# Seven block products for the first layer of three quarters of a dense network, on one Trainium2 core

## The reference

```python
def _moe_ref(x, U, V, w_ch1, w_ch2):          # x: 2 x 768 x 512
    xt = x.transpose(0, 2, 1)
    h = xt @ U @ V
    u = x + h.transpose(0, 2, 1)
    ch = np.maximum(u @ w_ch1, 0.0) @ w_ch2   # 512 -> 2048 -> 512
    return u + ch
```

## Time and profile before

| | us |
|---|---|
| median of 3 runs | 510.38 |
| lowest, highest | 510.18, 510.39 |
| the profiled execution | 510.51 |
| its span, first to last instruction | 508.7 |
| TensorE busy | 501.7 |
| VectorE busy | 255.3 |
| ScalarE busy | 202.3 |
| GpSimd busy | 45.6 |

### The profile page before, as it was taken

How to read it: one execution, slowest core, us unless ns; L and a number is a source line. 1 busy time by engine, 2 the same in 40 slices (tenths; PEclk the granted TensorE clock), 3 DMA queues, 4 the chain that set the end, 5 groups by cost and what they waited for, 6 DMA issues and landing times.

```text
span 508.7 us, 8626 instructions
## 1 busy us (share of the span) xinstructions
PE 501.7 (99%) x3460; PEld 468.5 (92%) x3460; DVE 255.3 (50%) x594; ACT 202.3 (40%) x403; POOL 45.6 (9%) x65
## 2 busy tenths in 40 slices
PE   8899999999999999999999999999999999999997
PEld 7679999999999999999999999999889889989987
DVE  5776654655455345354453554785544643552501
ACT  6575531442433244241431413554723632551410
POOL 6693310301000000000000000000000000000000
PEclk9999999999999999999999999999999999999999
DMA  8998533112112022132231331300010000001001
GB/s 283 339 267 265 150 110 92 43 44 83 41 44 82 1 84 62 36 134 100 79 130 41 126 125 43 124 1 1 0 43 21 2 27 36 0 15 48 1 0 62
DMA packets 13127, 40.53 MB, mean 80 GB/s; under 512 B 1728, under 2 KB 2240, under 8 KB 13088
## 3 DMA queue, kind: packets, MB, share of 16 engines
q1 hardware_dynamic: 12656, 39.20, 24.0%
q10 hardware_dynamic: 432, 0.79, 0.4%
HBM read 36.84 MB, written 3.15 MB: 79 GB/s over the span
## 4 chain that ended last, share of the span: by engine, by line
PE 94%; DMA 3%; POOL 1%; DVE 0%; SPq 0%; issue 0%; POOLq 0%
PE ps L788 91%; DMA V<-in_V 3%; PE ps L843 2%; PE ps L791 1%; DMA vT<-in_vT 1%; POOL Vs L370 1%; POOL vwin L386 0%; DVE vsum L593 0%; POOL Vs L366 0%; SPq L245 0%; DVE scratch L781 0%; SPq L208 0%; SPq L220 0%; DVE mixr L626 0%; DVE mixr L624 0%
## 5 line engine op out<-in xcount | busy, mean ns | idle before, releaser
L788 PE MATMUL ps<-u_hi,w_hi 128*128 128x384 f32 x256 | 87.4, 341 | 0.0
L788 PE MATMUL ps<-h_hi,w_hi 128*128 128x384 f32 x256 | 87.1, 340 | 0.0
L788 PE MATMUL ps<-h_hi,w_lo 128*128 128x384 f32 x256 | 85.9, 335 | 0.0
L788 PE MATMUL ps<-h_lo,w_hi 128*128 128x384 f32 x256 | 85.9, 335 | 0.0
L788 PE MATMUL ps<-u_hi,w_lo 128*128 128x384 f32 x256 | 85.9, 335 | 0.0
L788 PE MATMUL ps<-u_lo,w_hi 128*128 128x384 f32 x256 | 85.8, 335 | 0.0
L507 ACT ACTIVATE h_hi<-ps 128x384 fp32r<-128x384 f32 x64 | 31.5, 492 | 118.2 <-PE ps L788 118.1
L704 DVE SCALAR_TENSOR_TENSOR h_lo<-ps,h_hi 128x384 fp32r<-128x384 f32 x64 | 35.7, 558 | 68.6 <-ACT h_hi L507 68.5
L709 DVE TENSOR_TENSOR yT<-ps,yT 128x384 f32<-128x384 f32 x64 | 35.6, 556 | 54.1 <-PE ps L788 54.1
L788 PEld LDWEIGHTS ps<-u_hi,w_hi 128*128 128x128 f32 x256 | 48.1, 188 | 1.8 <-issue 1.5
L788 PEld LDWEIGHTS ps<-h_hi,w_hi 128*128 128x128 f32 x256 | 48.0, 188 | 1.5 <-issue 1.5
(11 more groups left out here) (96 smaller groups left out, 752.2 us busy)
## 6 DMA issues: line engine op xcount, KB each, us to landing
wraw<-in_w SPq DMA_DIRECT2D x42, 512.0 KB, 3.5
vwin<-in_vw SPq DMA_DIRECT2D x7, 580.5 KB, 13.1
kT<-in_kT SPq DMA_DIRECT2D x8, 400.0 KB, 8.8
vT<-in_vT SPq DMA_DIRECT2D x8, 384.0 KB, 10.0
out<-scratch SPq DMA_DIRECT2D x11, 256.0 KB, 2.0
qt<-in_qT SPq DMA_DIRECT2D x6, 384.0 KB, 11.7
vwin<-in_vw SPq DMA_DIRECT2D x1, 387.0 KB, 8.4
qt<-in_qT ACTq DMA_DIRECT2D x1, 384.0 KB, 7.0
```

The costliest lines, as they stand in the source:

```text
L788: return nc.tensor.matmul(o, lhsT, rhs, start=start, stop=stop)
```

## The change

Quarters 5, 6 and 7 do the first layer by Strassen's scheme in Winograd's form. The hidden block pair and the feature pairs make a 2x2 block matrix of the weights (feature halves i by hidden halves f, blocks of 256x256), the features and token chunks a 2x2 block matrix of u. Seven products of blocks take the place of eight. For each j (0, 1: the 128-wide half of a hidden block) there is one pair index m = 2(Q-5) + j and seven products, each of 6 matmuls 128x384, in the order P1, P6, P7, P5, P2, P4, P3, in banks 3 to 7 in turn.

- GpSimd forms four sums of u (T1 to T4, 128x768) after u is complete, and for each fast quarter four sums of w1 (S1 to S4, 128x512) from `wraw`. High and low halves of these: ScalarE and VectorE (`high_t`, `low_t` at g = 4, 6 of Q=4; `high_s`, `low_s` at g = 12, 13 of Q=4 and after the drains of k = 3, 5 of the second layers).
- VectorE forms seven sums from the products' banks (x, y, c22, z, c11, c21, c12), ScalarE copies P1 out. The hidden rows come from SBUF sums: h rows 0, 1 from c11, 2, 3 from c21, 4, 5 from c12, 6, 7 from c22. ScalarE writes all high halves; low halves of c11 and c21 are VectorE's, of c22 and c12 GpSimd's, in two instructions each.
- The second layer keeps its 96 matmuls; its first group waits for the low halves of c11 and c21.
- SyncE's w2 parts of quarters 5 to 7 wait for the third and fourth sum of GpSimd. The m2 parts are spread anew: two in Q=4, two in Q=5, none in Q=6, two in Q=7's second layer, four in the final stage's first eight groups.
- Buffers for the sums lie over those of the attention; m2's buffers are in two pieces.

```diff
@@ -40,7 +40,12 @@
...
-PARTS_LAST = [(1, "w2", 0), (3, "w2", 1), (4, "m2", 0), (6, "m2", 1), (7, "m2", 2), (9, "m2", 3)]
+S1, S3, S2, S4 = range(4)
+T1, T2, T4, T3 = range(4)
+NP = 7
+P1, P6, P7, P5, P2, P4, P3 = range(NP)
+LATE_AT = [0, 1, 4, 5]
+PREV_W2 = [-2, -4, -1, 0, 1, 2, 3, 5]
 UX_SLOT, XV_SLOT = 50, [52, 56]
@@ -179,14 +201,31 @@
         def parts_before(b, Q):
-            return 4 * Q + 2 if b == 0 else 6 * Q - 6
+            return 4 * Q + 2 if b == 0 else (18, 24, 30, 34)[Q - 4]
@@ -280,13 +319,14 @@
                 n += 1
                 load_part(n, src)
             for r in range(NQ):
-                last = r == NQ - 1
                 parts = [w2_part(r, 0), w2_part(r, 1)]
-                parts += [m2_part(m) for m in (range(2 * r, 2 * r + 2) if not last else range(6, 10))]
-                if not last:
+                parts += [m2_part(m) for m in ((0, 1), (2, 3), (), range(4, 10))[r]]
+                if r < NQ - 1:
                     parts += [w1_part(r + 1, a) for a in range(2)]
-                for src in parts:
+                for j, src in enumerate(parts):
                     n += 1
+                    if r > 0 and j < 2:
+                        sp.wait_ge(s_step, 4 * (r - 1) + 3 + j)
                     load_part(n, src)
             out_rows = out.rearrange("b s c -> (b s) c")
@@ -430,6 +470,56 @@
...
+                nc.gpsimd.tensor_tensor(two(t_sum, n, CH), a, b, op).then_inc(t_step, 1)
+            def u_block(i, c):
+                return yT[:, 1, 2 * i:2 * i + 2, 1 + CH * c:1 + CH * c + CH]
+            pool.wait_ge(yt_done, 16)
+            pool.wait_ge(ulo_done, 12)
+            t_add(T1, u_block(0, 1), u_block(0, 0), ALU.subtract)
+            pool.wait_ge(t_step, 1)
+            t_add(T2, u_block(1, 1), two(t_sum, T1, CH), ALU.subtract)
+            pool.wait_ge(t_step, 2)
+            t_add(T4, u_block(1, 0), two(t_sum, T2, CH), ALU.subtract)
+            t_add(T3, u_block(1, 1), u_block(0, 1), ALU.subtract)
+            def s_add(n, a, b, op):
+                nc.gpsimd.tensor_tensor(two(s_sum, n, 256), a, b, op).then_inc(s_step, 1)
+            def w_sums(q):
+                def w_block(i, f):
+                    return wraw[:, i, :].rearrange("p (t n) -> p t n", t=2)[:, :, 256 * f:256 * f + 256]
+                n = parts_before(1, Q=5 + q)
+                pool.wait_ge(w_in[0], 8 * n)
+                pool.wait_ge(w_in[1], 8 * n)
+                if q == 0:
+                    pool.wait_ge(tlo_done, 2)
+                need(pool, slo_done, 2 * q)
+                s_add(S1, w_block(0, 1), w_block(1, 1), ALU.add)
+                s_add(S3, w_block(0, 0), w_block(0, 1), ALU.subtract)
+                pool.wait_ge(s_step, 4 * q + 1)
+                s_add(S2, two(s_sum, S1, 256), w_block(0, 0), ALU.subtract)
+                pool.wait_ge(s_step, 4 * q + 3)
+                s_add(S4, w_block(1, 0), two(s_sum, S2, 256), ALU.subtract)
+            def low_relu(row, src, order, m, done):
+                pool.wait_ge(hb_done, 4 * m + order)
+                nc.gpsimd.tensor_scalar(src, src, 0.0, None, ALU.max).then_inc(relu_sums, 1)
+                pool.wait_ge(relu_sums, 2 * m + (1 if order == 1 else 2))
+                nc.gpsimd.tensor_tensor(h_lo[:, row, :], src, h_hi[:, row, :].bitcast(f32), ALU.subtract).then_inc(done, 1)
+            w_sums(0)
+            for q in range(3):
+                for j in range(2):
@@ -528,15 +618,10 @@
...
+                        high_t((g - 4) // 2)
+                    if b == 1 and g in (12, 13):
+                        high_s(0, g - 12)
             def mix_scale(b, c, p, n):
@@ -555,14 +640,71 @@
                     if p > DC * i:
                         mix_high(p - 1, n0 + p - 1)
+            def high_t(i):
+                act.wait_ge(t_step, 2 * i + 2)
+                nc.scalar.activation(t_hi[:, 2 * i:2 * i + 2, :], t_sum[:, 2 * i:2 * i + 2, :], ACT.Copy).then_inc(thi_done, 1)
+            def high_s(q, i):
+                act.wait_ge(s_step, 4 * q + 2 * i + 2)
+                act.wait_ge(pr_done, 14 * q)
+                nc.scalar.activation(s_hi[:, 2 * i:2 * i + 2, :], s_sum[:, 2 * i:2 * i + 2, :], ACT.Copy).then_inc(shi_done, 1)
+            def high_part(Q, i, kind, j):
+                n = parts_before(1, Q) + i + 1
+                act.wait_ge(w_in[(n - 1) % 2], 16 * ((n + 1) // 2))
+                nc.scalar.activation(part_dst(kind, j, 1, Q, True), wraw[:, (n - 1) % 2, :], ACT.Copy).then_inc(whi_done, 1)
+            def relu_sum(row, src):
+                nc.scalar.activation(h_hi[:, row, :], src, ACT.Relu).then_inc(hb_done, 1)
+            def fast_quarter(Q):
+                q = Q - 5
+                for j in range(2):
+                    m = 2 * q + j
...
+                    need(act, c11_sum, m)
+                    nc.scalar.activation(summed("p1"), p_bank(m, P1), ACT.Copy).then_inc(p1_copied, 1)
+                    if j == 0:
+                        high_part(Q, 0, "w2", 0)
+                    elif Q == 5:
+                        high_part(Q, 2, "m2", 0)
+                    act.wait_ge(c22_sum, m + 1)
+                    relu_sum(6 + j, summed("c22"))
+                    act.wait_ge(c11_sum, m + 1)
+                    relu_sum(j, summed("c11"))
+                    if j == 0:
+                        high_part(Q, 1, "w2", 1)
+                    elif Q == 5:
+                        high_part(Q, 3, "m2", 1)
+                    act.wait_ge(c21_sum, m + 1)
+                    relu_sum(2 + j, summed("c21"))
+                    act.wait_ge(c12_sum, m + 1)
+                    relu_sum(4 + j, summed("c12"))
+                if Q < 7:
+                    for i in range(2):
+                        high_part(Q, (4 if Q == 5 else 2) + i, "w1", i)
+                    for i in range(2):
+                        high_s(q + 1, i)
@@ -727,13 +871,84 @@
...
+            def low_relu(row, src, order, m, done):
+                dve.wait_ge(hb_done, 4 * m + order)
+                nc.vector.scalar_tensor_tensor(out=h_lo[:, row, :], in0=src, scalar=0.0, in1=h_hi[:, row, :].bitcast(f32),
+                                               op0=ALU.max, op1=ALU.subtract).then_inc(done, 1)
...
+            def add_to(out, product, other, m, done):
+                dve.wait_ge(pr_done, NP * m + product + 1)
+                nc.vector.tensor_tensor(summed(out), p_bank(m, product), summed(other), ALU.add).then_inc(done, 1)
+            def fast_quarter(Q):
+                q = Q - 5
+                for j in range(2):
+                    m = 2 * q + j
+                    dve.wait_ge(p1_copied, m + 1)
+                    need(dve, h11_done, m)
+                    add_to("x", P6, "p1", m, x_sum)
+                    if j == 0:
+                        low_part(Q, 0, "w2", 0)
+                    elif Q == 5:
+                        low_part(Q, 2, "m2", 0)
+                    dve.wait_ge(x_sum, m + 1)
+                    need(dve, h21_done, m)
+                    add_to("y", P7, "x", m, y_sum)
+                    dve.wait_ge(y_sum, m + 1)
+                    need(dve, h22_done, m)
+                    add_to("c22", P5, "y", m, c22_sum)
+                    need(dve, h12_done, m)
+                    add_to("z", P5, "x", m, z_sum)
+                    dve.wait_ge(z_sum, m + 1)
+                    add_to("c11", P2, "p1", m, c11_sum)
+                    dve.wait_ge(c22_sum, m + 1)
+                    add_to("c21", P4, "y", m, c21_sum)
+                    low_relu(j, summed("c11"), 2, m, h11_done)
+                    add_to("c12", P3, "z", m, c12_sum)
+                    low_relu(2 + j, summed("c21"), 3, m, h21_done)
+                    if j == 0:
+                        low_part(Q, 1, "w2", 1)
+                    elif Q == 5:
+                        low_part(Q, 3, "m2", 1)
+                for k in range(8):
+                    c, d = divmod(k, DC)
+                    dve.wait_ge(dense_done, 80 + 8 * q + k + 1)
+                    nc.vector.tensor_tensor(x_out(1, d, c), bank(BANK[8 + k], CH), x_out(1, d, c), ALU.add).then_inc(drained, 1)
+                    if Q < 7:
...
+                        if k in (0, 2):
+                            low_part(Q, (4 if Q == 5 else 2) + k // 2, "w1", k // 2)
+                        if k in (3, 5):
+                            low_s(q + 1, (k - 3) // 2)
+                    else:
+                        for p in (k,) if k < 7 else (7, 8):
+                            if p < 8:
+                                mix_add(0, 0, p, p)
+                            if p > 0:
+                                mix_low(p - 1, p - 1)
+                        if k in (1, 4):
@@ -756,12 +971,15 @@
             for Q in range(NQ):
                 quarter(0, Q, PARTS_B0)
-            for Q in range(NQ, 2 * NQ):
-                quarter(1, Q, PARTS_B1 if Q < 7 else PARTS_LAST)
+            quarter(1, 4, PARTS_B1)
+            for Q in range(5, 8):
```

(75 more changed lines are left out.)

85 lines of the change are left out of this document (64 added, 21 removed).

## The result

The changed kernel takes 509.44 us (median of 12 runs, 508.43 to 513.02), beside 510.99 of the kernel before on the same chips (12 runs, 510.18 to 513.14): a ratio of 0.9972, 95% interval 0.9959 to 0.9986, some 1.5 us or 0.3% faster. Repeated with 12 more runs it was 0.9980 (0.9965 to 0.9994). The forecast was 506.1, 4.3 us faster. The sign was right, the size nearly three times too large.

A forecast was written before the change was run, and what follows sets the result against it. TensorE, busy 99% of the span, was taken as the bound. Removed matmuls 6.24, less stalls 1.68 and final-stage lag 0.15, gave 4.41 us off the profiled 510.51: 506.1 us, range 504.1 to 510.0.

The forecast's parts named there:

- The saving: First layers of Q=5 to 7: 84 matmuls instead of 96 each, at 0.1733 us, 6.24 us less.
- The place of the stall: One TensorE gap of 0.5 to 0.7 us a quarter, at the second layer's first matmul; none at P6.
- I take 0, the row's own behaviour, and keep the other end: VectorE starting during GpSimd work: cost per meeting 0 to 0.93 us, taken as 0 from a copy at 59.02 us.
- the walk: Operation-by-operation timing of the product pairs: stalls 1.68 us before the second layers; total 504.7 to 507.5 us, chance 0.56.
- the second: VectorE waits 0.46 us at each operation with two SBUF inputs: 509.2 us; chance 0.23 including mild forms of late sums.
- The third: VectorE and GpSimd exclude each other wholly in the product pairs, bounding TensorE through the banks: 517.0 us; chance 0.08.
- The fourth: GpSimd's s sums late at P6, 2.4 us each instead of 1.2: 512.6 us; chance 0.05 in full.
- the fifth: TensorE loses an interval to waits at each of 42 products, 7.1 us, nothing left: 513 us; chance 0.02.
- the first: Handovers cost nothing or the timing of the pairs is too slow: 504.1 us, the floor; chance 0.06.
- Handovers: From the end of a VectorE operation to the restart of a stalled TensorE's matmul: 0.29 us.
- GpSimd's durations: GpSimd low half in the pairs: max of some 0.45 us plus 0.93 subtraction, 1.5 with the handover.
- The final stage: Four m2 parts in its first 8 groups: lag 3.8 against 3.6 us slack at second value group, costing 0.15.

The follow-up runs named there:

- both edits: Changed kernel plus GpSimd's second-pair low halves waiting for VectorE's c11 half and second-layer hidden rows in order 0, 2, 1, 3: 505.97 us, 0.9904.

## Why the prediction was right or wrong

**The saving: right.** 36 matmuls of 0.1733, 6.24 us, are gone, and where nothing else waits (Q=6, both edits) 14.59 stands for 16.64.

**The place of the stall: right.** One wait a quarter, at the second layer's first matmul, released by VectorE's low half; no stall at a product, none at P6 (the second s half ends at 240.28 and 272.39, wanted near 242.4 and 274.9), none through the four late parts.

**Its size: wrong, and this is the step that failed.** The sum had 0.72 + 0.48 + 0.48 = 1.68; it is 1.23 + 1.34 + 1.35 = 3.92, 2.24 more. The failing step is the sentence on VectorE beginning while GpSimd is at work, "I take 0, the row's own behaviour, and keep the other end". In the row at 59 us VectorE came first. When it comes second, it waits: in Q=6 and Q=7 the half of c11 comes second, because GpSimd's c22 subtraction has just begun, and in Q=5 the weight parts ahead of it do. The runs price it: 0.65 in Q=5 (15.79 to 15.14 without GpSimd's halves), 0.80 and 0.81 in Q=6 and 7 (15.90 and 15.91 to 15.10 with GpSimd moved behind), 2.26 in all. What is left is 0.58, 0.54 and 0.54, 1.66, against the walk's 1.68. That the sums agree to 0.02 is luck (the walk had 0.72, 0.48 and 0.48, 0.14 too much in Q=5 and 0.06 too little twice), but no quarter is off by more than 0.14. The walk was sound; a known unknown was entered at its cheap end, 0, where the other end that the prediction names, 0.93, was near the 0.8 measured. In Q=5 the meetings lie earlier, at the parts (VectorE, then GpSimd):

```profile
249.50 0.73 DVE L898 SCALAR_TENSOR_TENSOR h_lo<-c_sum,h_hi 128x384 fp32r<-128x384 f32 x1
250.16 1.52 DVE L892 TENSOR_TENSOR w_lo<-wraw,w_hi 128x1024 fp32r<-128x1024 f32 x1
251.61 0.54 DVE L903 TENSOR_TENSOR c_sum<-ps,c_sum 128x384 f32<-128x384 f32 x1
252.07 1.57 DVE L892 TENSOR_TENSOR m2a_lo<-wraw,m2a_hi 128x1024 fp32r<-128x1024 f32 x1
253.57 2.66 DVE L903 TENSOR_TENSOR c_sum<-ps,c_sum 128x384 f32<-128x384 f32 x5
256.36 0.56 DVE L898 SCALAR_TENSOR_TENSOR h_lo<-c_sum,h_hi 128x384 fp32r<-128x384 f32 x1
...
250.08 1.19 POOL L511 TENSOR_SCALAR c_sum<-c_sum 128x384 f32<-128x384 f32 x1 [0.26 <-ACT h_hi L658]
251.35 1.22 POOL L513 TENSOR_TENSOR h_lo<-c_sum,h_hi 128x384 fp32r<-128x384 f32 x1
```

The two parts take 1.52 and 1.57, not 1.22, and the half of c21 ahead of them 0.73; counted from the start of Q=5, the half of c11 at 256.36 comes 0.64 later than in the kernel without GpSimd's halves. The second part waited to near the end of GpSimd's subtraction (252.57). The first came 0.08 after the start of a max of 1.19 and lost only 0.30. So beside a max the wait is not its whole length, and it is the same each time: over the ten traces 31 operations of VectorE came early in a max, and all really began 0.80 to 0.81 us before its end, 0.35 to 0.39 after its start, while ten that came later than that lost nothing. Why a max lets go so early is open.

**The rivals.** The measured 509.44 stands next to the 509.2 of the second, and that is luck. It had the mechanism, VectorE waiting, and the wrong place for it: I charged it to VectorE's total, which gave 3.1 in Q=5 and nothing in Q=6 and 7 because there was time to spare. But the price is paid by the one operation that TensorE waits for, or by those right ahead of it in VectorE's order, spare time or not, so that it is nearly even over the quarters (0.65, 0.80, 0.81). The third, full exclusion bounding TensorE through the banks, did not come. Between two-input operations the exclusion is nearly whole, but GpSimd is idle when most of VectorE's come, and the PSUM adds don't meet it. The fourth (late sums), the fifth (intervals lost at the products) and the first (504.1) are out.

**Handovers.** Forecast 0.29 from the end of VectorE to TensorE's matmul; measured 0.25, and then another 0.08 to the second matmul of the row. Three times 0.08 are the 0.25 of the repeated profile that the sum did not have; the first profile's 0.49 has intervals longer by some 0.0013 us through the second layers of Q=6 and Q=7 besides.

**GpSimd's durations.** "a max of some 0.45 (from the cast)" was far too low (min/median/max in ns over the changed kernel):

```profile
L511 POOL TENSOR_SCALAR c_sum<-c_sum x12: 1165/1168/2256, 247.1 to 323.4; 128x384 f32<-128x384 f32 x12
...
L513 POOL TENSOR_TENSOR h_lo<-c_sum,h_hi x12: 1012/1201/1572, 248.4 to 324.6; 128x384 fp32r<-128x384 f32 x12
```

A max of 128x384 takes 1.17, 2.26 when VectorE holds it up. The h12 rows had time for it, but it also moved GpSimd's subtraction under the half of c11. An estimate from the rows of Q=6: with a max of 0.45 from 286.85 and the same 0.08 between the two, the subtraction would have run from 287.38 to 288.39, and the half of 288.18 would have lost some 0.07 and not 0.79. So two terms failed together in Q=6 and Q=7: the wait that was put at nothing, and the duration that brought the meeting about. No run separates them, as none has a shorter max.

**The final stage.** Forecast: lag 3.8 against 3.6 of slack, 0.15. VectorE's second s half for Q=5 and for Q=6, ScalarE's last copy of the first chunk and its first gates in the changed kernel:

```profile
239.07 1.21 DVE L886 TENSOR_TENSOR s_lo<-s_sum,s_hi 128x1024 fp32r<-128x1024 f32 x1
...
271.17 1.22 DVE L886 TENSOR_TENSOR s_lo<-s_sum,s_hi 128x1024 fp32r<-128x1024 f32 x1 [0.69 <-ACT s_hi L650]
...
360.59 0.53 ACT L711 ACTIVATE h_hi<-scratch 128x384 fp32r<-128x384 f32 x1 [0.71 <-DVE scratch L984]
...
368.50 1.09 ACT L717 ACTIVATE scratch<-ps 128x512 f32<-128x512 f32 x2
```

The final stage began 1.09 earlier, so the copy (358.44 in the earlier trace rows) would be due at 357.35 and came at 360.59: lag 3.24. The gates come as much later. It stayed inside the slack, and no gap stands at the second value group: the 0.15 did not come. The 0.26 of the first profile is spread over many intervals, and the repeated one has 0.00.

**The contention rule of the Trainium skill** (GPSIMD Engine Reference, Key points): VectorE and GpSimd contend where VectorE has two SBUF inputs. The runs agree, and they add what the prediction left open, as that section does not say who waits: it holds in both directions, the second to come waits for the one under way (2.25 for 1.17 on GpSimd, 1.35 for 0.56 on VectorE), up to 0.14 us before the end of a subtraction. Where both start within 0.01 us of each other (a max at 282.69, a part at 282.70), GpSimd is the one that waits.

## What to carry to other kernels

Where a term of the sum has no row in one direction, look at which operation of the new order stands in that direction just before the bounding engine's wait, and price it there at its full size; an average over an engine's spare time hides it. When GpSimd helps VectorE, order its work behind the VectorE operation that the critical wait hangs on, not only by when its inputs are ready: here that one wait was worth 1.6 us, as much as the change had brought. And a wait that is "just met" behind another is the next bound as soon as the first is gone.
